# Batch loops written out, and a new order for the first batch of an attention + two-layer MoE kernel

## The reference, cut to what matters

```python
# 1. chunked attention: batch 4, heads 8, sequence 768, head size 64; 8 memory keys per head
for c in range(24):                      # chunks of 32 queries
    k_full = concat(mem_k, k[c*32-16 : c*32+40])      # clipped at the sequence's ends
    a = softmax(q[chunk] @ k_full.T / 8)
    out[chunk] = a @ v_full
x = out as [3072 tokens, 512]
# 2. SoLU layer, w_in [512, 1024], w_out [1024, 512]
h = x @ w_in
solu = h * softmax(h)
x = ((solu - mean) / sqrt(var + 1e-6) * g_ln) @ w_out
# 3. hard-swish layer, [512, 2048] and [2048, 512]
h = x @ w_in2
out = (h * clip(h + 3, 0, 6) / 6) @ w_out2
```

## Time and profile before

| | before |
|---|---|
| median of 3 runs | 946.51 us |
| profiled execution | 949.08 us, span 947.3 us |
| busy PE / DVE / ACT / POOL | 902.4 / 674.4 / 471.2 / 268.6 us |
| mean granted TensorE clock | 0.976 of full speed |
| span up to `attend` of tile 6 (end of step kk = 0 of batch 1) | 81.59 us |

### The profile page before, as it was taken

The page is one execution under the profiler, slowest core; times in us unless marked ns, Lnnn a source line. Parts: engine busy times, 40 slices in busy tenths (PEclk is TensorE's granted clock), DMA queues, the critical chain, the costliest instruction groups (busy, mean ns, idle before and its releaser), DMA issues.

```text
span 947.3 us, 17198 instructions
## 1 busy us (share of the span) xinstructions
PE 902.4 (95%) x6124; PEld 807.5 (85%) x6124; DVE 674.4 (71%) x1097; ACT 471.2 (50%) x1092; POOL 268.6 (28%) x334
## 2 busy tenths in 40 slices
PE   6879999699997999999999999999999899999998
PEld 5768988589895888889978888888789899999997
DVE  3996878578774677857686555545777978878783
ACT  4675555355554565644675554555653333333320
POOL 3473355435331153462002332323540000000000
PEclk8999999799997999999999999999999999999999
DMA  9643365426743467359573333332987335344441
GB/s 183 143 117 82 79 179 168 153 59 158 221 137 104 100 180 199 122 154 329 190 256 118 127 133 133 129 137 106 341 323 265 117 109 157 97 149 123 140 140 45
DMA packets 146935, 146.84 MB, mean 155 GB/s; under 512 B 96936, under 2 KB 107176, under 8 KB 145832
## 3 DMA queue, kind: packets, MB, share of 16 engines
q1 hardware_dynamic: 133267, 100.29, 36.5%
q0 software_dynamic: 7920, 38.94, 11.7%
q10 hardware_dynamic: 5669, 6.56, 2.1%
HBM read 90.05 MB, written 55.71 MB: 154 GB/s over the span
## 4 chain that ended last, share of the span: by engine, by line
PE 85%; DVE 5%; DMA 5%; issue 3%; ACT 1%; POOL 0%; ACTq 0%; SPq 0%; DVEq 0%; POOLq 0%
PE banks L975 27%; PE banks L1240 23%; PE banks L1023 22%; PE banks L920 3%; PE banks L966 3%; PE banks L928 3%; PE banks L890 2%; PE banks L949 2%; DMA gs_raw<-g_scratch 2%; PE banks L990 1%; DMA ws<-w_split_scratch 1%; DMA xs_raw<-x_scratch 1%; DVE gs_raw L1878 1%; DVE prob L1586 1%; DVE gs L1547 1%
## 5 line engine op out<-in xcount | busy, mean ns | idle before, releaser
L1240 PE MATMUL banks<-vs,gs 128*128 128x256 f32 x2016 | 244.5, 284 | 3.6 <-DVE o_stage L1911 2.9
L1240 PEld LDWEIGHTS banks<-vs,gs 128*128 128x128 f32 x2016 | 243.7, 193 | 4.4 <-DVE o_stage L1911 3.1
L1023 PE MATMUL banks<-xs,ws 128*128 128x512 f32 x1008 | 231.3, 390 | 3.3 <-DMA ws<-w_split_scratch 2.3
L1023 PEld LDWEIGHTS banks<-xs,ws 128*128 128x128 f32 x1008 | 188.2, 188 | 45.0 <-DMA ws<-w_split_scratch 3.2
L1507 ACT CAST gs<-gs_raw 128x1792 fp32r<-128x1792 f32 x48 | 81.4, 1695 | 133.6 <-DVE gs_raw L1878 133.5
L975 PE MATMUL banks<-y_t,w_out 128*128 128x384 f32 x768 | 140.8, 338 | 0.0
L975 PEld LDWEIGHTS banks<-y_t,w_out 128*128 128x128 f32 x768 | 132.2, 188 | 0.7
L975 PE MATMUL banks<-w_in,x_t 128*128 128x512 f32 x504 | 122.5, 399 | 0.0
L975 PEld LDWEIGHTS banks<-w_in,x_t 128*128 128x128 f32 x504 | 94.8, 192 | 20.2
L1298 ACT ACTIVATE prob<-score,small 96x128 f32<-96x128 f32 x256 | 99.3, 392 | 18.7 <-DVE small L1564 17.8
L1878 DVE TENSOR_TENSOR gs_raw<-gs_raw 128x256 f32<-128x256 f32 x192 | 82.6, 431 | 31.6 <-DMA gs_raw<-g_scratch 26.6
(11 more groups left out here) (94 smaller groups left out, 1078.2 us busy)
## 6 DMA issues: line engine op xcount, KB each, us to landing
g_scratch<-part SPq DMA_DIRECT2D x96, 256.0 KB, 2.0
gs_raw<-g_scratch SPq DMA_DIRECT2D x45, 512.0 KB, 3.9
q_in<-in_q_dram SPq DMA_DIRECT2D x32, 192.0 KB, 4.1
x_scratch<-x_out ACTq DMA_DIRECT2D x32, 192.0 KB, 3.5
out_dram<-o_stage SPq DMA_DIRECT2D x12, 512.0 KB, 5.5
k_in<-in_k_dram SPq DMA_DIRECT2D x24, 240.0 KB
v_in<-in_v_dram SPq DMA_DIRECT2D x24, 240.0 KB
v_split_scratch<-v_split POOLq DMA_DIRECT2D x3, 1792.0 KB, 7.8
```

The lines of the kernel that those rows point to most:

```text
L1023: mm = pe.matmul(ps, ws[:, W_OF[i], a, kc, :], xs[g][X_OF[i]][:, m, kc, :], start=(fresh and x == 0), stop=(x == len(passes) - 1), skip_gr ...
L1240: mm = pe.matmul(m_ps[i][:, s, :], gs[x][:, a, G_OF[i], s * P:(s + 1) * P], vs[p][:, m, V_OF[i], :], start=(p == 0 and s == 0 and y == 0), ...
```

## The change

Three things are done. (1) `Fori` over the batches becomes a Python loop on SP, PE, ACT and DVE, so that the code of three batches stands one behind the other. (2) `first_batch()` has a new order on PE, ACT, DVE, POOL and SP, and takes in step kk = 0 of batch 1: scores of tile 7, `hidden` of m-tile 3, `turn_ln` of m-tile 2, `attend` of tile 6. The batch behind it begins with kk = 1 (`start=1`). The 12 identity matmuls of `keep_busy(6)` (6 calls, 12 instructions in the trace) go. (3) POOL requests w_in pieces 0 and 1 straight behind the masks, and `g_ln` behind piece 2. The diff, cut to its core (the lists of ACT and DVE are cut to their ends):

```diff
     load_q(0, 2)
     load_k(0, 2)
     load_q(0, 3)
-    load_k(0, 3)
     load_v(0, 0)
     load_v(0, 1)
+    load_k(0, 3)
     load_q(0, 4)
     load_k(0, 4)
     load_q(0, 5)
+    load_k(0, 5)
     load_v(0, 2)
     load_v(0, 3)
-    load_k(0, 5)
     load_q(0, 6)
+    load_k(0, 6)
     load_v(0, 4)
-    load_k(0, 6)
+    load_q(0, 7)
     load_v(0, 5)
-    load_q(0, 7)
     load_k(0, 7)
     load_v(0, 6)
...
-with sp.Fori(1, B) as b:
+for b in range(1, B):
...
 def load_weights(p):
-    if p < 2:
-        pool.wait_ge(k_in_here[0], kv_here(0, 0))
-    else:
+    if p >= 2:
         pool.wait_ge(w_raw_here[p % 2], 16 * (p // 2))
...
-        pool.wait_ge(y_turned, 2 * (m - 1))
+        pool.wait_ge(y_turned, {2: 2, 3: 6}[m])
...
 def first_batch():
-    pool.wait_ge(k_in_here[0], kv_here(0, 0))
-    with nc.allow_non_contiguous_dma(reason="one vector, once"):
-        pool.dma_start(g_ln, moe_g_ln.rearrange("(c p) -> p c", p=P)).then_inc(g_ln_here, 16)
     load_weights(0)
     load_weights(1)
     high_weights(0)
     load_weights(2)
+    load_gain()
     high_weights(1)
     load_weights(3)
     high_weights(2)
     high_weights(3)
     load_weights(4)
     scale_weights(4)
-    load_weights(5)
-    scale_weights(5)
     high_weights(4)
     low_weights(4, 0)
+    load_weights(5)
+    load_weights(6)
     low_weights(4, 1)
     root_of(0)
-    load_weights(6)
+    scale_weights(5)
+    normal_of(0)
+    low_weights(4, 2)
+    high_weights(5)
     load_weights(7)
-    normal_of(0)
+    low_weights(4, 3)
     scale_weights(6)
-    low_weights(4, 2)
-    low_weights(4, 3)
-    high_weights(5)
-    low_weights(5, 0)
-    scale_weights(7)
     high_weights(6)
-    low_weights(5, 1)
     root_of(1)
     normal_of(1)
+    low_weights(5, 0)
+    low_weights(5, 1)
     low_weights(5, 2)
+    scale_weights(7)
     low_weights(5, 3)
+    low_weights(6, 0)
     high_weights(7)
-    low_weights(6, 0)
     low_weights(6, 1)
-    root_of(2)
-    normal_of(2)
     low_weights(6, 2)
     low_weights(6, 3)
     low_weights(7, 0)
+    root_of(2)
     low_weights(7, 1)
+    normal_of(2)
     low_weights(7, 2)
     low_weights(7, 3)
+    root_of(3)
+    normal_of(3)
...
-        pe.wait_ge(x_lo_done, m + 2)
+        pe.wait_ge(x_lo_done, TPG * (m // MPG) + m % MPG + 2)
...
     turn_k(1, early_ps[1])
     scores(1, False)
+    turn_half(0, 0)
     pe.wait_ge(qk_copied, 3)
     turn_q(2, early_ps[0])
     pe.wait_ge(qk_copied, 4)
     turn_k(2, early_ps[1])
+    turn_half(0, 1)
+    scores(2, False)
+    pe.wait_ge(prob_copied, 1)
+    turn_half(1, 0)
+    attend(0, 0, True)
     pe.wait_ge(qk_copied, 5)
     turn_q(3, early_ps[0])
-    turn_half(0, 0)
-    scores(2, False)
-    turn_half(0, 1)
+    pe.wait_ge(prob_copied, 2)
+    turn_half(1, 1)
     pe.wait_ge(qk_copied, 6)
     turn_k(3, early_ps[1])
-    attend(0, 0, True)
-    pe.wait_ge(prob_copied, 1)
-    turn_half(1, 0)
-    keep_busy(6)
-    pe.wait_ge(prob_copied, 2)
-    turn_half(1, 1)
     attend(0, 1, False)
     scores(3, False)
     pe.wait_ge(qk_copied, 7)
     hidden_part(0, 0)
-    hidden_part(0, 1)
     pe.wait_ge(prob_copied, 3)
     turn_half(2, 0)
+    hidden_part(0, 1)
     pe.wait_ge(qk_copied, 8)
     hidden_part(0, 2)
-    hidden_part(0, 3)
     pe.wait_ge(prob_copied, 4)
     turn_half(2, 1)
+    hidden_part(0, 3)
     pe.wait_ge(prob_copied, 5)
     turn_q(4, turn_ps[0])
-    attend(0, 2, False)
     pe.wait_ge(prob_copied, 6)
     turn_k(4, turn_ps[1])
+    attend(0, 2, False)
     pe.wait_ge(qk_copied, 9)
     turn_half(3, 0)
     scores(4, False)
+    pe.wait_ge(qk_copied, 10)
+    turn_half(3, 1)
     pe.wait_ge(prob_copied, 7)
     turn_q(5, turn_ps[0])
     hidden_part(1, 0)
     hidden_part(1, 1)
     hidden_part(1, 2)
-    pe.wait_ge(qk_copied, 10)
-    turn_half(3, 1)
-    hidden_part(1, 3)
     pe.wait_ge(prob_copied, 8)
     turn_k(5, turn_ps[1])
+    hidden_part(1, 3)
     attend(0, 3, False)
+    scores(5, False)
     pe.wait_ge(qk_copied, 11)
     turn_half(4, 0)
-    scores(5, False)
     pe.wait_ge(qk_copied, 12)
     turn_half(4, 1)
     pe.wait_ge(prob_copied, 9)
...
     scores(6, False)
     pe.wait_ge(qk_copied, 14)
     turn_half(5, 1)
+    attend(0, 5, False)
     pe.wait_ge(prob_copied, 11)
     turn_ln_half(1, 0)
+    hidden_part(3, 0)
     pe.wait_ge(prob_copied, 12)
     turn_ln_half(1, 1)
-    attend(0, 5, False)
-
-def batch(b, last=False):
-    for kk in range(TILES):
+    hidden_part(3, 1)
+    hidden_part(3, 2)
+    pe.wait_ge(y_lo_done, 3)
+    turn_q(7, turn_ps[0])
+    pe.wait_ge(y_lo_done, 4)
+    turn_k(7, turn_ps[1])
+    hidden_part(3, 3)
+    scores(7, False)
+    pe.wait_ge(qk_copied, 15)
+    turn_half(6, 0)
+    pe.wait_ge(qk_copied, 16)
+    turn_half(6, 1)
+    pe.wait_ge(prob_copied, 13)
+    turn_ln_half(2, 0)
+    pe.wait_ge(prob_copied, 14)
+    turn_ln_half(2, 1)
+    attend(0, 6, False)
+    pe.wait_ge(y_lo_done, 5)
+    pe.wait_ge(y_lo_done, 6)
...
+batch(1, start=1)
+for b in range(2, B):
     batch(b)
...
     copy_q(1, early_ps)
     copy_k(1, early_ps)
     exp_half(0, 0)
+    exp_half(0, 1)
+    copy_half(0, 0)
     copy_q(2, early_ps)
-    exp_half(0, 1)
     copy_k(2, early_ps)
-    act.wait_ge(prob_turned, 1)
     exp_half(1, 0)
-    copy_half(0, 0)
+    act.wait_ge(prob_turned, 2)
+    exp_half(1, 1)
     copy_half(0, 1)
-    act.wait_ge(scores_done, 6)
+    act.wait_ge(prob_turned, 3)
+    exp_half(2, 0)
     copy_q(3, early_ps)
-    exp_half(1, 1)
     high_x(0, 0, 0)
+    act.wait_ge(av_done, 1)
     copy_half(1, 0)
...
     copy_q(7, turn_ps)
     copy_k(7, turn_ps)
-
-def batch(b, last=False):
-    for kk in range(TILES):
+    copy_half(6, 0)
+    copy_half(6, 1)
+    high_ln_half(2, 0)
+    high_ln_half(2, 1)
+    exp_half(7, 0)
+    high_x(6, 2, 1)
+    exp_hidden(3)
+    exp_half(7, 1)
+    copy_q(8, turn_ps)
+    copy_k(8, turn_ps)
...
     mask_half(0, 0)
+    max_half(0, 0)
     mask_half(0, 1)
-    max_half(0, 0)
-    low_weights(0)
     max_half(0, 1)
     den_half(0, 0)
+    rec_half(0, 0)
+    scale_half(0, 0)
     mask_half(1, 0)
-    rec_half(0, 0)
-    max_half(1, 0)
-    scale_half(0, 0)
     den_half(0, 1)
     mask_half(1, 1)
     rec_half(0, 1)
+    scale_half(0, 1)
+    max_half(1, 0)
     max_half(1, 1)
-    scale_half(0, 1)
+    low_weights(0)
     den_half(1, 0)
     rec_half(1, 0)
+    mask_half(2, 0)
+    scale_half(1, 0)
+    max_half(2, 0)
+    mask_half(2, 1)
+    den_half(1, 1)
     low_weights(1)
-    scale_half(1, 0)
-    mask_half(2, 0)
-    max_half(2, 0)
-    den_half(1, 1)
+    rec_half(1, 1)
+    den_half(2, 0)
+    scale_half(1, 1)
+    rec_half(2, 0)
     low_x(0, 0, 0)
-    rec_half(1, 1)
-    scale_half(1, 1)
-    mask_half(2, 1)
+    scale_half(2, 0)
     low_weights(2)
+    low_x(1, 1, 0)
     max_half(2, 1)
...
+    mask_half(7, 0)
+    max_half(7, 0)
+    mask_half(7, 1)
+    low_ln_half(2, 0)
+    low_ln_half(2, 1)
+    max_hidden(3)
+    max_half(7, 1)
+    low_x(6, 2, 1)
+    den_hidden(3)
+    den_half(7, 0)
+    rec_half(7, 0)
+    scale_half(7, 0)
+    rec_hidden(3)
+    den_half(7, 1)
+    rec_half(7, 1)
+    scale_half(7, 1)
+    solu_of(3)
+    stats_of(3)
+    mean_of(3)
+    moments_of(3)
```

More of the change, by code:

```diff
@@ L592, in load_weights, with load_gain @@
                 pool.dma_start(dst, src).then_inc(w_raw_here[p % 2], 16)
+            def load_gain():
+                with nc.allow_non_contiguous_dma(reason="one vector, once"):
+                    pool.dma_start(g_ln, moe_g_ln.rearrange("(c p) -> p c", p=P)).then_inc(g_ln_here, 16)
             def scale_weights(p):
@@ L810, in mix_ws, with batch @@
                     nc.gpsimd.tensor_tensor(ws_raw[:, to, :], ws_raw[:, a, :], ws_raw[:, b, :], op).then_inc(wt_done, 1)
-            def batch(b, last=False, steps=None, tokens=False):
+            def batch(b, last=False, steps=None, tokens=False, start=0):
                 for kk in range(TILES):
@@ L817, in batch @@
                         load_tokens(1, 1)
-                    if w["mm1"]:
+                    if w["mm1"] and kk >= start:
                         normalise(MPG * (i - 1) + u, u)
@@ L831, in _ @@
             first_batch()
-            batch(1, steps=0)
+            batch(1, steps=0, start=1)
             batch(2, steps=TILES)
@@ L1134, in first_batch, with batch @@
                 turn_half(5, 1)
+                attend(0, 5, False)
                 pe.wait_ge(prob_copied, 11)
                 turn_ln_half(1, 0)
+                hidden_part(3, 0)
                 pe.wait_ge(prob_copied, 12)
                 turn_ln_half(1, 1)
-                attend(0, 5, False)
-            def batch(b, last=False):
-                for kk in range(TILES):
+                hidden_part(3, 1)
[17 more added lines that the diff above has]
+                pe.wait_ge(y_lo_done, 6)
+            def batch(b, last=False, start=0):
+                for kk in range(start, TILES):
                     w = work(kk, last)
@@ L1172, in _ @@
             first_batch()
```

(37 more changed lines are left out.)

69 lines of the change are left out of this document (27 added, 42 removed).

## The result

| | before | after |
|---|---|---|
| median of the runs on the same chip | 946.77 us (4 runs) | 917.42 us (4 runs, 916.04 to 919.6) |
| profiled execution / span | 949.08 / 947.3 us | 916.04 / 914.1 us |
| mean granted clock | 0.976 | 0.991 |
| `attend` of tile 6 (end of kk = 0 of batch 1) starts at | 81.59 us | 73.81 us |
| `attend` of kk = 7 of batch 1 | 172.71 us | 166.19 us |

The ratio of after to before is 0.9681, 95% interval 0.9644 to 0.9717: 29.35 us less by the medians, where 28.1 were forecast (918.4 us). The work is the same (DVE and ACT are busy as long as before); PE is busy 13.3 us less because fewer of its matmuls run at half clock, 12 identity matmuls being gone as well.

A forecast was written before the change was run, and what follows sets the result against it. PE was taken to bound the seven-step stretches, with long stalls at the loops' jumps between batches. Loops 22.6 plus first batch 5.5 (1.1 + 5.6 - 1.2) gave 28.1 us, so 946.51 became 918.4 us, range 912.5 to 926.5.

The forecast's parts named there:

- (1): Steps from kk = 7 to kk = 0 between batches: writing out the loops on four engines saves 12.24 + 10.36, together 22.6 us.
- front, up to the maximum of m-tile 0: Start of batch 1: the new order brings DVE's maximum of m-tile 0 from 37.54 to about 36.4, gain 1.1 us.
- m-tiles 1 and 2: Batch 1 up to 69.17 us: DVE full in both orders with the same instructions, distance from m-tile 0 kept, 0.
- kk = 0: wait and clock: Step kk = 0 of batch 1: `hidden_part(3, 0)` to `(3, 2)` fill PE's 3.74 us idle, clock stays (1.9 us): 5.6 us.
- loss behind it (low part, SoLU of m-tile 3): Behind the new kk = 0: late low part of m-tile 2's `y_t` 0.6 us, SoLU of m-tile 3 0.6, loss 1.2 us.
- code supply, POOL's work, load order: Longer straight code, POOL's second-layer weight work losing cover, and SP's later `load_k(0, 3)`: each priced at 0.
- (3): Start of batch 1: weight requests go out 5.2 us earlier, at best ending DVE's 2.92 us wait; k window loss 0.
- `keep_busy`: Front of batch 1: dropping 12 matmuls priced at 0; by the skill's rule (2) and (3) would sum near 3 us.
- B: First batch: new order brings nothing, only the loops count, 923.9 us, or 926.9 with the k window's 3 us; chance 0.19.
- C: First batch: comes to DVE's floor, low part for kk = 1 at 68.4 against 78.4, total 913.9 us; chance 0.11.
- D: Steps between batches: stops belong only in part to the jump, half of 22.6 stays, 929.6 us; chance 0.05.
- E: kk = 1 to 7 of batches 2 and 3: longer code not supplied in time, twelve stops cost 41 us, 959; chance 0.04.
- F: Whole kernel: next to no effect, PE's time only shifted into a later wait, 946.5 us; chance 0.03.

The follow-up runs named there:

- experiment 1: The kernel before with only the four batch loops of PE, ACT, DVE and SP written out, old first batch kept: 922.95 us, ratio 0.9722.
- experiment 7: The changed kernel with the first two w_in pieces again waiting for the k window of tile 0: 916.03 us, ratio 0.9648.
- experiment 11: The changed kernel with identity matmuls added in four of PE's waits in the first 25 us: 914.89 us, ratio 0.9639.

## Why the prediction was right, point by point

By the starts of `attend` in the two profiles:

| term | forecast | measured |
|---|---|---|
| (1) steps into batches 2, 3 and last | 22.6 us | 12.65 + 10.92 + 0.60 = 24.2 us; 24.15 with the loops alone |
| front, up to the maximum of m-tile 0 | 1.1 us | 37.54 - 36.48 = 1.06 us |
| m-tiles 1 and 2 | 0 | 1.67 us, in part work moved out of the stretch |
| kk = 0: wait and clock | 5.6 us | 5.05 us |
| loss behind it (low part, SoLU of m-tile 3) | -1.2 us | -1.04 us in kk = 1; another -0.22 in kk = 4 goes with the loops |
| code supply, POOL's work, load order | 0 | 0.2 us, the shorter seven steps of batches 2 and 3 |
| up to the last batch | 28.1 us | 30.9 us |

The forecast for the median was nearer (918.4 against 917.42 us) than its terms: by the profiles 2.8 us were missed, of which (1) makes 1.6 and the m-tiles 1.67, while kk = 0 gave 0.55 less than forecast. The two profiled executions stand at the two far ends, 949.08 being above the median before and 916.04 the lowest of the four after, and by the medians 29.35 us are gained. That the median came out within 1 us is in part luck.

- **What bounds.** Shown: the straight stretches did not change, and experiment 1 took the long steps away without touching anything else.
- **(1)** was right in mechanism, a little small. The term mis-sized is the measure: 11.21 us, the step at the loop's exit, still held 0.6 us that went with the loop; the true straight step is 10.65 us (10.77 would have been nearer). That ACT's and DVE's jumps stop PE as well was read from PE's second idle times, and half wrong: alone, DVE's shows no cost and ACT's 0.6 us. The sum did not depend on it, since all loops go. Of the Trainium skill's section that I cited ("Runtime: NRT & Kernel Launch", "Instruction fetch mechanics") the rule on taken branches fits the steps with PE's jump (16.33 us against 10.65), and its small cost of crossing a block of code fits the straight stretches of 91.0 us. Its larger code memory for PE, from which I drew that PE's jump might be free, did not make it so: PE's is the dear one. Whether a batch of PE's code fits in that memory no run here shows.
- **(3)** the size 0 for the k window was right (PE takes k at 6.97 us after, 6.77 before, by its own timelines; 6.34 to 7.35 in the nine profiles with the new order). The gain laid to the early pieces was not: with the new lists the wait of 2.92 us goes without them (experiment 7), and what else they bring is below the spread.
- **Front, 1.1 us.** The number came out, but not as a fixed gain. The maximum of m-tile 0 starts at 34.6 to 37.8 us in the nine profiles with the new order (36.2 in the mean), at 37.4 and 37.5 in the two with the old: a gain of 1.3 us in the mean, and anything from -0.3 to 2.9 in one profile. Part of the swing is the clock: where the first scores run at full clock (1.12 us) the first mask comes at 8.9 to 9.6 us instead of 10.5 to 11.3. The profile of the changed kernel was one of those, so of its 1.06 us the order can't claim all. But two profiles with the late first mask have `attend` of tile 6 at 73.50, before its 73.81, so this is not all of the swing. The walk kept the clock of rows 8 and did not foresee that the new order holds it at half for 10 to 17 us where the old one has 7. One of the prediction's own signs of being wrong, a clock of 0.5 beyond 30 us, was just met: it rises at about 30.2 (0.94 in the mean of 30 to 32 us).
- **m-tiles 1 and 2.** Here the step failed that said DVE is full in both orders, its instructions are the same, and so the m-tiles keep their distance. From maximum to maximum it was 11.79 and 11.32 us; it is 11.00 and 10.44, in every profile with the new lists within 0.05. The instructions between the maxima are not the same. Before (first two lines) and after, from the maximum of m-tile 0 to that of m-tile 2:

```profile
L1586 DVE TENSOR_TENSOR prob<-prob,small 96x512 f32<-96x512 f32 x6 | 4.9, 821 | 0.1
L1547 DVE TENSOR_TENSOR x_t<-banks,x_t 128x384 fp32r<-128x384 f32 x3 | 1.6, 546 | 0.0
L1620 DVE TENSOR_TENSOR prob<-prob,small 96x512 f32<-96x512 f32 x4 | 2.6, 680 | 0.0
L1581 DVE TENSOR_TENSOR x_t<-banks,x_t 128x384 fp32r<-128x384 f32 x2 | 1.1, 554 | 0.1
```

The new list has `scale_half(3, 0)` ahead of the first of these maxima and `scale_half(5, 1)` and `low_x(4, 0, 1)` behind the last. DVE is busy for 22.46 us in this stretch before and 19.97 after; two divisions (`scale_half`), two `rec_half`, one `den_half` and one `low_x`, 2.4 us at their shortest, are most of that, and 0.8 us more of waiting takes a part back. So part of the 1.67 us is work done elsewhere: in front, where DVE had waited (23.51 us busy instead of 21.66 up to the first maximum), and in kk = 0. The rows of the front, of the m-tiles and of kk = 0 are therefore not three separate effects; their sum, 7.8 us up to tile 6, is what the marks measure.
- **kk = 0.** `hidden` of m-tile 3 took the place of the idle time, as forecast; 0.67 us before `hidden_part(3, 0)` and 0.24 before `turn_ln` are new short waits. The loss of 1.2 us is nearly there: kk = 1 takes 14.30 us against 13.26 (0.95 is the wait at 75.64). Step kk = 4 takes 0.22 us more too (10.99 us), but not by the new first batch: it takes 10.98 us in experiment 1, with the old one.
- **`keep_busy`.** Priced at nothing, and putting it back shows no effect that stands out of the spread. The Trainium skill's rule in "TensorE: Matmul & The Clock Gate" (Part 1), by which I had the gain near 3 us, is not borne out for these twelve, but it points the right way: identity matmuls in four of PE's waits keep the clock (experiment 11).
- **Rivals.** B (the first batch brings nothing) falls with 6.77 us, though its sign, a slower clock in front, did come; C (DVE's floor, 68.4 us for the low part) was not reached, it ends at 75.4; D falls with experiment 1; E with the straight stretches of 91.0 us, F with the time itself.

## What to carry to other kernels

Measure a loop's jump where the trace has the same step with and without it, and count the slow clock behind the stop as part of its price. Before writing a loop out on every engine, look which engine bounds: here PE's jump alone costs 5.7 us where one jump on all four costs 8.3. A gain read from one profile of a start-up stretch, in which PE waits often, has to be set beside the spread of several profiles. And where an order changes, compare two marks only after counting what stands between them in either list.

## What the runs showed of the hardware

- One jump back on PE, in a batch of some 770 matmuls and as many weight loads: 3.17 us stopped and 2.5 us more busy time at half clock. On DVE (about 155 instructions a batch) and on SP the step takes 10.66 and 10.63 us, as without the jump; on DVE a stop of up to about 2 us would be hidden beneath its wait of 2.15 us.
- Costs of jumps do not simply add: 5.7 (PE) and 0.6 (ACT) alone, 8.3 us for all four together.
- The granted clock of nearly the same list of instructions differs in the first 32 us from execution to execution: PE's first scores, at about 8 to 9 us, take 1.12 or 2.02 us, and the last rise to full clock comes between about 27 and 32 us. `attend` of tile 6 moves too, 71.89 to 75.11 us over nine profiles, partly with the clock; from the maximum of m-tile 0 to that `attend` all nine take 37.3 us, and the later stretches are not moved either.
